# Attention on 96 partitions of six tokens, with 64-row score tiles and 512-byte operand placing, ahead of an expert layer and an MLP

## The reference

```python
def sm_attn(qq, kk, vv):
    a = softmax(scale * qq @ kk.T)       # over the keys
    return a @ vv
p_packed = sm_attn(p, k, v)              # 32 rows a head
out = sm_attn(q, p_packed, p_packed)     # 576 rows a head
x = out.transpose(0, 2, 1, 3).reshape(B * S, H * D)

P = exp(x @ w_gate - max); 8 times: rows, then columns divided by their sums, times N / E
y = sum over 8 experts e of P[:, e] * (relu(x @ w1[e]) @ w2[e])      # 512 -> 1024 -> 512

h = relu(y @ w_in);  result = (s * h * h + b) @ w_out                # 512 -> 2048 -> 512
```

## Time and profile before

| | |
|---|---|
| median of 3 runs | 1781.79 us (1780.3 to 1781.91) |
| the profiled execution | 1782.02 us, its span 1780.1 us |
| PE busy | 1753.5 us (99%) |
| PE weight load (PEld) | 1519.3 us (85%) |
| DVE busy | 932.5 us (52%) |
| ACT busy | 724.0 us (41%) |
| POOL busy | 625.9 us (35%) |
| read from HBM, written | 73.16 MB, 4.72 MB |
| packets under 512 bytes | 43744 of 97294 |

### The profile page before, as it was taken

One profiled execution on the slowest core, in us unless ns is written; L12 is line 12 of the kernel. 1 busy time (PEld: TensorE's weight loads), 2 busy tenths in 40 slices (PEclk: granted clock), 3 DMA queues, 4 the chain that ended last, 5 costly groups with the idle time before them and its releaser, 6 DMA issues.

```text
span 1780.1 us, 26764 instructions
## 1 busy us (share of the span) xinstructions
PE 1753.5 (99%) x9861; PEld 1519.3 (85%) x9861; DVE 932.5 (52%) x1441; ACT 724.0 (41%) x1606; POOL 625.9 (35%) x400
## 2 busy tenths in 40 slices
PE   7899999999999999999999999999999999999999
PEld 5688888888898889888888988898888888888887
DVE  5755654444544444554455445544546555555555
ACT  4564446444345434544443444345443222222222
POOL 1264444434534444344444434434431001111100
PEclk9999999999999999999999999999999999999999
DMA  9811112111111211111121111111100000000002
GB/s 211 175 48 36 36 45 51 36 48 35 36 36 35 59 35 47 35 35 35 35 49 45 35 47 35 35 35 38 44 24 24 13 25 24 24 24 24 0 0 106
DMA packets 97294, 78.50 MB, mean 44 GB/s; under 512 B 43744, under 2 KB 84704, under 8 KB 97248
## 3 DMA queue, kind: packets, MB, share of 16 engines
q1 hardware_dynamic: 97248, 77.89, 18.1%
HBM read 73.16 MB, written 4.72 MB: 44 GB/s over the span
## 4 chain that ended last, share of the span: by engine, by line
PE 95%; DVE 3%; ACT 1%; SPq 1%; DMA 0%; issue 0%; DVEq 0%
PE PS L1121 94%; PE PS L1139 1%; SPq L361 1%; DVE acc L977 1%; PE PS L1377 0%; DMA k_raw<-k_dram 0%; DVE gate L954 0%; ACT first_raw L546 0%; DVE a_parts L857 0%; ACT a_parts L546 0%; DVE stat L808 0%; DVE stat L833 0%; DVE gate L940 0%; DVE pp L822 0%; SPq L364 0%
## 5 line engine op out<-in xcount | busy, mean ns | idle before, releaser
L1121 PE MATMUL PS<-w_hi,h_hi 128*128 128x512 f32 x1440 | 563.7, 391 | 1.5 <-DVE acc L977 1.5
L1121 PE MATMUL PS<-w_lo,h_hi 128*128 128x512 f32 x1440 | 562.4, 391 | 0.0
L1121 PE MATMUL PS<-w_hi,h_lo 128*128 128x512 f32 x1440 | 562.0, 390 | 0.0
L982 DVE SCALAR_TENSOR_TENSOR acc<-PS,gate,acc 128x512 f32<-128x512 f32 x504 | 378.0, 750 | 267.1 <-PE PS L1121 267.1
L683 ACT ACTIVATE h_hi<-PS 128x576 fp32r<-128x576 f32 x256 | 167.1, 653 | 674.9 <-PE PS L1121 674.2
L1121 PE MATMUL PS<-a_parts,g_parts 128*128 128x288 f32 x3072 | 437.7, 295 | 0.8 <-DVE h_lo L963 0.6
L1121 PEld LDWEIGHTS PS<-a_parts,g_parts 128*128 128x128 f32 x3072 | 417.9, 188 | 6.1 <-DVE h_lo L963 1.1
L546 ACT ACTIVATE g_raw<-PS 32x256 f32<-32x256 f32 x992 | 373.2, 376 | 14.2 <-PE PS L1121 0.3
L963 DVE SCALAR_TENSOR_TENSOR h_lo<-PS,h_hi 128x576 fp32r<-128x576 f32 x256 | 194.0, 758 | 327.6 <-ACT h_hi L683 327.6
L1121 PEld LDWEIGHTS PS<-w_hi,h_hi 128*128 128x128 f32 x1440 | 270.3, 188 | 60.9 <-DVE acc L977 4.0
L1121 PEld LDWEIGHTS PS<-w_hi,h_lo 128*128 128x128 f32 x1440 | 270.3, 188 | 57.8
(11 more groups left out here) (129 smaller groups left out, 1111.1 us busy)
## 6 DMA issues: line engine op xcount, KB each, us to landing
stage<-moe_w_dram SPq DMA_DIRECT2D x96, 512.0 KB, 5.0
out_dram<-acc SPq DMA_DIRECT2D x18, 256.0 KB, 2.0
k_raw<-k_dram SPq DMA_DIRECT2D x16, 256.0 KB, 6.0
q_raw<-q_dram SPq DMA_DIRECT2D x16, 256.0 KB, 5.6
v_raw<-v_dram SPq DMA_DIRECT2D x4, 1024.0 KB, 6.4
stage<-moe_w_in_dram SPq DMA_DIRECT2D x16, 256.0 KB, 2.8
stage<-moe_w_out_dram SPq DMA_DIRECT2D x8, 512.0 KB, 3.4
k_tail<-k_dram SPq DMA_DIRECT2D x4, 128.0 KB, 5.0
```

The lines of the kernel that those rows point to most:

```text
L982: return nc.vector.scalar_tensor_tensor(out=dst, in0=y, scalar=share, in1=dst, op0=ALU.mult, op1=ALU.add)
L1121: return nc.tensor.matmul(dst, lhsT, rhs, start=start, stop=stop)
```

## The change

The attention is laid out anew; the expert layer and MLP keep every instruction.

- A batch's 576 tokens are 96 partitions (`TOK`) of six (`RUN`). `load` fetches keys, queries or values of four heads in one transfer, whose runs are six tokens, 1536 bytes. There is no tail. k, q and v take two transfers each in a batch, where they took five, five and two; the packed queries come in two transfers for each batch (`p_twice`, each twice side by side) where one served all four.
- A unit turns two tokens of a head (`turn_heads`): four transposes of 96 x 128, so that on rows 0 to 63 stands one token's 64 numbers and on rows 64 to 127 the other's. There are six such units for k and for q, three for e and for a.
- Products over 64 numbers use half the rows of the array each: `scores1` is 8 products of 288 columns a quad (4 heads by 2 halves, each 64 rows by 32 array columns), `scores2` 144 products of 32 columns for each of three chunks of 192 tokens, the gates 8 of 8 columns. `packed` has 48 products with the values, over 96 rows, in place of 40.
- The zero blocks go, and with them `blockmask`, `odd_even`, `queries_by_head`; `packed_values` has two copies instead of five, `lo_of_packed` one instruction instead of four. `off_max2`, `exp2`, `inverse2` and `normalise2` work on three chunks of 96 x 512 instead of five of up to 128 x 256.
- `scores2` has one pair of banks outside the last batch: a chunk waits until the one before has been taken.
- Expert 0's first weights are loaded after batch 3's keys (b == 1 in the loop) instead of after batch 2's.
- Output rows are scattered by `by_run`, so a tile of 128 rows is two transfers; their loop is written out.
- Two pads move the buffers. In the built program `w1_hi` and `w1_lo` began 128 bytes past a multiple of 512 and `a_parts`, `pp_parts`, `g_parts`, `w2_*`, `g_raw*`, `h_hi`, `h_lo`, `mlp_f` 320 bytes past one; all of them begin at a multiple of 512 now.

```diff
-    MAIN = 512
-    TAIL = S - MAIN
-    CH = MAIN // P
-    CHUNKS = [(c * P, P) for c in range(CH)] + [(MAIN, TAIL)]
-    NC = len(CHUNKS)
+    TOK = 96
+    RUN = S // TOK
+    NC = RUN // 2
+    PAIR = 2 * TOK
+    UNITS_IN = NC * 2
...
+        sb("to_512_bytes", [P, 96])
...
-        sb("to_64_bytes", [P, 22])
+        sb("to_512_bytes_again", [P, 102])
...
+        def scores2_of(b, c):
+            at = s2_bank(b, c) * BANK + BANK - H * NPACK
+            return PS[0:TOK, at:at + 2 * H * NPACK]
 
...
+            def runs(src, Q):
+                return src[Q * 4:Q * 4 + 4].rearrange("h (p c) d -> p h (c d)", c=RUN)
+
+            def load(dst, src, arrived):
+                for Q in range(QUADS):
+                    sp.dma_start(dst[0:TOK, Q * 4:Q * 4 + 4, :], runs(src, Q)).then_inc(arrived[Q], 16)
+
+            def load_queries(bb):
+                src = p[bb].rearrange("(u h) n d -> (h n) u d", h=4)
+                for twice in range(2):
+                    sp.dma_start(p_twice[bb % 2][:, :, twice, :], src).then_inc(p_in[bb % 2], 16)
+
+            def load_keys(bb):
+                load(k_raw[bb % 2], k[bb], k_in[bb % 2])
+                load_queries(bb)
...
+                sp.wait_ge(tr_full, UNITS.index(("q", b, UNITS_IN - 1)) + 1)
+                load(q_raw[0], q[b + 1], q_in)
                 sp.wait_ge(pp_full, b + 1)
-                load_values(b + 1)
+                load(v_raw, v[b + 1], [v_in, v_in])
                 if b + 2 < B:
-                    load(k_raw, b, k, k_in[b % 2], b + 2)
-                if b == 0:
+                    load_keys(b + 2)
+                if b == 1:
                     src1, src2 = expert_part(0, 0)
                     load_by_head(src1)
-                    load_w2(0, src2)
-                    sp.dma_start(s_and_b[:, 0:1], s_.rearrange("(o n) -> o n", o=1).to_broadcast([P, 1])
-                                 ).then_inc(sb_in, 16)
-                    sp.dma_start(s_and_b[:, 1:2], b_.rearrange("(o n) -> o n", o=1).to_broadcast([P, 1])
-                                 ).then_inc(sb_in, 16)
+            load_w2(0, src2)
+            sp.dma_start(s_and_b[:, 0:1], s_.rearrange("(o n) -> o n", o=1).to_broadcast([P, 1])
...
+            by_run = out.rearrange("(b p c) n -> b c p n", b=B, c=RUN)
+            sent = 0
+            for t in range(TILES):
+                sp.wait_ge(acc_done, (GROUPS - 1) * TILES + t + 1)
+                row = 0
+                for b, c, at, n in pieces_of_tile(t):
+                    sp.dma_start(by_run[b, c, at:at + n, :], acc[row:row + n, t, :]).then_inc(out_sent, 16)
+                    row += n
+                    sent += 1
+            sp.wait_ge(out_sent, 16 * sent)
...
-                src = full(unit)
-                copy(ppT[i][:], src.rearrange("p (j n) -> p j n", j=PAIRS))
-                for o in range(2):
-                    rows = slice(o * HALF, (o + 1) * HALF)
-                    for r in range(2):
-                        part = src[rows, :].rearrange("p (u x) -> p u x", u=QUADS)
-                        at = r * P + (2 * r + o) * NPACK
-                        last = copy(pp_parts[rows, 2 * r + o::4, b * NPACK:(b + 1) * NPACK],
-                                    part[:, :, at:at + NPACK])
-                last.then_inc(evacuated(unit), 1)
...
+                src = full(unit)[:, 0:QUADS * P]
+                copy(ppT[i][:], src)
+                copy(pp_parts[0:HALF, :, b * NPACK:(b + 1) * NPACK],
+                     src[0:HALF, :].rearrange("d (h n) -> d h n", n=NPACK)).then_inc(evacuated(unit), 1)
...
             def lo_of_packed(b):
-                i, unit = b % 2, UNITS.index(("pp", b, 0))
+                unit = UNITS.index(("pp", b, 0))
                 wait_evacuated(dve, [unit])
-                for o in range(2):
-                    rows, other = slice(o * HALF, (o + 1) * HALF), slice((1 - o) * HALF, (2 - o) * HALF)
-                    for r in range(2):
-                        hq = 2 * r + o
-                        nc.vector.tensor_tensor(
-                            pp_parts[other, hq::4, b * NPACK:(b + 1) * NPACK],
-                            ppT[i][rows, r::2, hq * NPACK:(hq + 1) * NPACK],
-                            pp_parts[rows, hq::4, b * NPACK:(b + 1) * NPACK].bitcast(F32),
-                            ALU.subtract).then_inc(pp_split, 1)
+                cols = slice(b * NPACK, (b + 1) * NPACK)
+                nc.vector.tensor_tensor(
+                    pp_parts[HALF:P, :, cols], ppT[b % 2][0:HALF, :].rearrange("d (h n) -> d h n", n=NPACK),
+                    pp_parts[0:HALF, :, cols].bitcast(F32), ALU.subtract).then_inc(pp_split, 1)
...
+            def turn_heads(what, b, n, raw, Q, c):
+                cols = slice(2 * c * D, (2 * c + 2) * D)
+                transposes(what, b, n, [(hq * TOK, raw[0:TOK, 4 * Q + hq, cols]) for hq in range(4)])
...
-                for o in range(2):
-                    lhsT, kk = pT[i][:, Q, o * HALF:(o + 1) * HALF], kT[i][:, 2 * Q + o, :]
-                    mm(bank(S1B)[o * HALF:(o + 1) * HALF, :], lhsT, kk[:, 0:MAIN])
-                    last = mm(bank(S1B + 1, TAIL)[o * HALF:(o + 1) * HALF, :], lhsT, kk[:, MAIN:S])
+                for hq in range(4):
+                    h, out_rows = 4 * Q + hq, slice(hq * NPACK, (hq + 1) * NPACK)
+                    for r in range(2):
+                        rows = slice(r * HALF, (r + 1) * HALF)
+                        last = mm(bank(S1B + r, SPAN)[out_rows, :], pT[i][rows, h * NPACK:(h + 1) * NPACK],
+                                  kT[i][rows, h, :])
                 last.then_inc(s1_full, 1)
...
+                    wait_evacuated(pe, range(LAST - 3, LAST))
+                elif b == B - 1 and c == 2:
                     pe.wait_ge(s2_taken, n - 1)
-                for Q in range(QUADS):
-                    for o in range(2):
-                        last = mm(bank(s2_bank(b, c))[0:rows, Q * P:(Q + 1) * P],
-                                  qT[i][:, 2 * Q + o, col:col + rows], ppT[i][:, 2 * Q + o, :], o == 0, o == 1)
+                elif n:
+                    pe.wait_ge(s2_taken, n)
+                for h in range(H):
+                    for r in range(2):
+                        rows = slice(r * HALF, (r + 1) * HALF)
+                        at = (s2_bank(b, c) + r) * BANK + (1 - r) * (BANK - H * NPACK) + h * NPACK
+                        for m in range(TOK // NPACK):
+                            toks = slice(m * NPACK, (m + 1) * NPACK)
+                            last = mm(PS[toks, at:at + NPACK],
+                                      qT[i][rows, h, c * TOK + m * NPACK:c * TOK + (m + 1) * NPACK],
+                                      ppT[i][rows, h * NPACK:(h + 1) * NPACK])
                 last.then_inc(s2_full, 1)
...
-                turn_a(b - 1, 4)
                 if final:
                     break
                 turn_k(b + 1, 3)
                 turn_k(b + 1, 4)
+                turn_k(b + 1, 5)
                 scores2(b, 0)
                 scores1(b + 1, 0)
+                turn_q(b + 1, 0)
                 scores2(b, 1)
-                turn_q(b + 1, 0)
-                scores2(b, 2)
                 turn_q(b + 1, 1)
-                scores2(b, 3)
+                turn_q(b + 1, 2)
                 packed_gates(b)
                 scores1(b + 1, 1)
-                turn_q(b + 1, 2)
-                scores2(b, 4)
                 turn_q(b + 1, 3)
+                scores2(b, 2)
                 turn_q(b + 1, 4)
+                turn_q(b + 1, 5)
```

More of the change, by code:

```diff
@@ L642, in _ @@
             exp1(0, 1)
-            for c in (2, 3, 4):
-                q_part(0, c)
+            for n in range(1, UNITS_IN):
+                q_part(0, n)
             for b in range(B):
-                i = b % 2
-                evacuate("e", b, 0, e1T[i][:, 0:CH, 0:P], chunks)
+                evacuate("e", b, 0, *turned_e(b, 0))
                 a_chunk(b - 1, 0)
@@ L692, in _ @@
             shift_first(2, 1, 0)
-            for c in range(4):
+            for c in range(2):
                 exp2(B - 1, c)
             relu(0, 0, 0, 0)
-            exp2(B - 1, 4)
+            exp2(B - 1, 2)
             shift_first(3, 0, 1, range(0, 4))
@@ L897, in _ @@
                 inverse1(b)
+                inverse2(b - 1, 2)
                 a_chunk(b - 1, 0)
-                evacuate("e", b, 1, e1T[b % 2][:, 0:CH, P:2 * P], chunks)
+                evacuate("e", b, 1, *turned_e(b, 1))
                 a_chunk(b - 1, 1)
-                inverse2(b - 1, 4)
                 a_chunk(b - 1, 2)
@@ L909, in _ @@
                     break
-                lo_of_packed(b)
                 off_max2(b, 0)
                 max1(b + 1, 0)
+                lo_of_packed(b)
+                inverse2(b, 0)
                 off_max2(b, 1)
-                inverse2(b, 0)
-                off_max2(b, 2)
+                max1(b + 1, 1)
                 inverse2(b, 1)
-                off_max2(b, 3)
```

(19 more changed lines are left out.)

345 lines of the change are left out of this document (143 added, 202 removed).

## The result

The changed kernel took **1804.2 us** (median of 4 runs, 1803.6 to 1805.2), the kernel before 1781.7 in the same comparison: ratio 1.0128 (95% interval 1.0113 to 1.0143), so 22.5 us slower. The prediction was 1756.6 us, with a range of 1728 to 1776: wrong in sign.

What follows compares the result with a forecast made beforehand. TensorE was taken to bound experts and MLP; in the attention TensorE, VectorE and DMA were all near full. 1782.0 less 20.1 (attention and end), 5.1 (padding) and 0.2 gave 1756.6 us, range 1728 to 1776.

Steps and rivals of the forecast that it cites:

- The padding: MLP's hidden products: operands at equal distance from a multiple of 512 bytes go from 233 to 227 ns, 5 us less.
- the kernel's end: Output's last tile: two transfers, the second issued after the first, lose 0.5 us.
- The rival of the absolute place: Outputs, hidden and MLP products: operands at 0 themselves quicken every pace, 39 us in place of 5, 1723 us; chance 0.15.
- GpSimd's split of the first weights: Expert 0's weights, loaded later: 7 us of splitting end at 57 us, ahead of batch 2's first normalise2 at 59; nothing waits.
- The cost of tiles: Attention on TensorE: 10 ns a scores2 pass, 0.6 us for scores1, at most 0.3 for gates, 1.7 for packed.
- VectorE's steps: Attention chain: reduction and subtraction of 512 scores 0.69 us each, with exp2 and normalise2 steps following.
- period of 17.0 us: Attention batches: VectorE's chain sets a period of 17.0 us instead of 21.3.
- The step that failed: TensorE's work in an attention batch: 3.8 us less, 14.9 us a batch, so TensorE stops being the bound if tiles overlap.
- The term of 7.3 us: Kernel's start: loads at 350 GB/s bring batch 0's scores2 at 20.3 us instead of 27.65, 7.3 us won.
- its lower end of 0.8: Kernel's start: if loads into 96 partitions stay at 221 GB/s, only 0.8 us is won; chance 0.13.
- Slower by placing: Outputs: operands at 0 fall to the slower 233 ns, 28 us lost while 20 are won, 1790 us; chance 0.09.
- Tiles do not overlap: scores2: 64-row tiles do not overlap or the array drains, 40 ns a pass, period about 24 us, 1776 us; chance 0.08.

Runs made afterwards that it cites:

- the last run of experiment 8: Changed kernel with scores2 in whole products of 96 tokens, thin filling (unread 128-column products) and loads into all 128 partitions: 1781.5 us, ratio 0.9993 to the kernel before.
- experiment 3: Changed kernel with each three scores2 products of 32 tokens made as one whole product of 96 tokens: 1791.7 us, ratio 1.0045 to the kernel before.
- (7): Changed kernel with SP waiting for each load of keys, queries or values to land before issuing the next: 1802.8 us, ratio 1.0129 to the kernel before.
- experiment 4: Kernel before with its scores2 products cut into tiles of 32 tokens, still 128 rows and the same loads: 1783.7 us, ratio 1.0008.
- (5): Changed kernel with whole scores2 products of 96 tokens, plus filling: unread 256-column products ahead of key and query units: 1785.4 us, ratio 1.0026 to the kernel before.
- experiment 6: Changed kernel, scores2 still in tiles of 32 tokens, plus thin filling (unread 128-column products ahead of units): 1812.3 us; with whole products of 96 tokens instead, 1785.7 us.
- (8): Changed kernel with keys, queries and values loaded into all 128 partitions, 4/3 of the bytes: 1802.4 us, ratio 1.0120 to the kernel before.
- experiment 1: Changed kernel with the two pads put back as in the kernel before: 1817.4 us, ratio 1.0198 to the kernel before.

## Why the prediction was wrong

**The padding and the kernel's end: right.** (`_hi` and `_lo` are the two parts into which a number is split; a product of the expert layer and the MLP is made as hi times hi, hi times lo and lo times hi.) The MLP's hidden products went from 233 to 227 ns, 5.1 us, as forecast:

```profile
1500.93 0.39 PE L1094 MATMUL PS<-a_parts,w_hi 128*128 128x512 f32 x1
1501.15 0.39 PE L1094 MATMUL PS<-g_parts,w_hi 128*128 128x512 f32 x1
1501.38 0.39 PE L1094 MATMUL PS<-a_parts,w_lo 128*128 128x512 f32 x1
1501.61 0.39 PE L1094 MATMUL PS<-a_parts,w_hi 128*128 128x512 f32 x1
```

Beside it the outputs' mean went from 228.5 to 227.7 ns (4320 x 0.8 = 3.3 us), and `hidden` from 132.35 to 132.75 (1.2 us lost). The rival of the absolute place fell with the result itself: everything stands at 0 and no pace fell below 227 ns. The end lost 0.7 us (0.5 forecast). Between batch 3's first `scores2` and the first output 1.4 us were lost, where 1.0 should have been won. GpSimd's split of the first weights stood at 81.3 to 88.2 us, ahead of a `normalise2` at 100.7, so nothing waited for it.

**The cost of tiles and of VectorE's steps: right, and beside the point.** 10.6 ns a pass in `scores2` (10 taken), 0.72 us for `scores1` (0.6), 0.3 to 0.4 for the gates (0.3), 1.55 for `packed` (1.7). VectorE's, ScalarE's and GpSimd's steps, by form up to 165 us:

```profile
L831 DVE TENSOR_REDUCE stat<-PS 96x16 f32<-96x512 f32 x12 | 8.1, 673 | 14.7 <-PE PS L1094 14.7
...
L519 POOL TENSOR_TENSOR second<-second,stat 96x512 f32<-96x512 f32 x6 | 6.5, 1087 | 36.4 <-DVE stat L845 36.4
...
L832 DVE TENSOR_TENSOR second<-PS,stat 96x512 f32<-96x512 f32 x6 | 4.1, 686 | 0.2
...
L621 ACT ACTIVATE acc<-acc 96x512 f32<-96x512 f32 x6 | 3.8, 630 | 15.4 <-DVE acc L832 15.4
```

These are 0.67, 0.69, 0.63 and 1.09 us, where the sum had 0.69, 0.69, 0.62 and 1.23. Yet the period of 17.0 us that they make never came, because TensorE did not do its share in the time put down.

**The step that failed** is "In sum ... 14.9 us a batch: TensorE stops being the bound if the tiles overlap". They do overlap, and the 14.9 us are about right for the passes alone: in the last run of experiment 8 a period at full clock has 19.1 us of TensorE, of which 2.6 are filling and some 1.5 the price of whole products. But the step counts passes and their durations at full clock, and leaves out two supplies:

- *Instructions.* 144 small products of `scores2` in place of 20 large ones are seven times the instructions in less time. Boundaries of 256 instructions now cost some 26 us ahead of the first output. Going from 1015 to 630 a batch gave back 12.5 us (experiment 3). The loads are part of it: while they are on their way a block is issued only 3.8 to 7.5 us after TensorE has gone on, and pacing them shortens the long stalls (7). I had priced them as a gain alone. Whether the longer runs make it worse isn't shown: experiment 4 has at most 3.6 us behind 256-byte runs, but the kernel before has 6.3 (boundary passed at 66.6, block issued at 72.9, with queries and values on their way). It cost nothing there, because the next boundary came only at 83.3.
- *The clock.* I took it as 1.00 because the earlier trace rows has it so, without asking what the removed zero blocks did for it. They were work of 128 rows on 128 columns. With them gone the lower level held for 58 us of the records, with stalls (the change) and nearly without (experiment 3). Useless products of 128 rows bring the clock back and the time down (5), and in the kernel before, with 128 rows in `scores2`, it stays up even in tiles of 32 (4). That it is the rows, and not the columns or the amount of work, no run separates. The trace of before had shown the engine at 0.86 from 6 to 18 us, while it was busy for 9.2 of 12 us.

The two are apart: filling alone leaves the stalls (`scores2` in tiles, experiment 6), whole products alone leave the clock (3).

**Start.** The term of 7.3 us was mis-sized, and its lower end of 0.8 as well. I took 350 GB/s "since the row of 1024-byte runs is nearest"; the loads came at 259 into 96 partitions, and at 391 into 128 (8). The first keys were there at 5.6 us (5.3 forecast), the packed queries of batch 1 at 22.5, and TensorE stood 2.8 us for them, since their turn is ahead of the second `e` unit. From there to `scores2` it took 8.5 us, where I had allowed 2.7 to 3.9: the sum let that chain run beside the loads, but in TensorE's order it stands behind them. The clock has its part in it too: up to 27.8 us the work of this chain takes some 2.5 us longer than the same transposes and `packed` take later at the upper level (an estimate from their durations; `packed` 2.19 us at 26.36, 1.55 at 53.16). The result is 31.0 us instead of 27.65, a loss of 3.4.

**The rivals.** "Slower by placing" named the sign and no more: no pace of 512 columns rose in the steady part. "Tiles do not overlap" is refuted by 10.6 ns. None held instructions or clock, and all the chance for slower (0.10) rested on wrong mechanisms.

What stays open: why the loads into unpadded places are slower (227 GB/s in the one profile of experiment 1, 259 to 276 in five with the padded places), and whether they are what cost the other 6 us there; why the outputs gained without moving; and how much of the whole loss is the clock alone, since it acts together with the stalls. With stalls, clock and the width of loads mostly out of the way the kernel stands at 1781.5 us, 9 us of filling included. The 1756.6 of the forecast was not reached by any version, and none had small tiles, no stalls and the upper level of the clock together, so what VectorE's chain alone would have made of the period is not shown.

## What to carry to other kernels

Cutting TensorE's work into many small products can move its limit from the array to the supply of instructions: count instructions a microsecond, not only passes, and look for "issue" waits in the middle of runs of equal products that stand 256 instructions apart. Work that looks useless, such as zeros that are multiplied, may be what keeps the clock up; when work is taken off TensorE, check the granted clock of the new kernel first, and by the durations of equal products where the records have not begun. Place both operands of a long stream at the same distance from a multiple of 512 bytes: here this alone gave 0.5%, and no version with the new attention was as fast.

## What the runs showed of the hardware

- Blocks of 256 TensorE instructions came 3.5 to 4.2 us apart at best; with loads on their way a boundary cost up to 6.7 us.
- Tiles of 64 rows by 32 columns: 10.6 ns a pass, three row pairs and column tiles side by side. The same product as 64 rows by 96 columns: 46 ns a pass (1.48 us for 32), so that fewer instructions cost TensorE 0.5 us a chunk.
- In "whole" the clock fell with TensorE busy for 4.75 of the 5.24 us before, and later stayed at its lower level while TensorE was busy for 24.4 of 25 us; its products were transposes and tiles of 64 rows.
- Loads into 96 partitions: 259 GB/s; into 128: 391.
- Distance of the operands modulo 512 bytes, for the MLP's hidden products of 512 columns: 0 gives 227 ns, 256 gives 228.5, 192 gives 233, 64 gives 236.
